# Outputs beside the next unit's state products, running sums after the second products, k and q in two sets of buffers

## What is computed

```python
f = 1.0 / (1.0 + np.exp(-f_logit))
for t in range(S):
    state = f[:, :, t, :, None] * state + np.einsum('bhd,bhe->bhde', k[:, :, t], v[:, :, t])
    y[:, :, t] = np.einsum('bhd,bhde->bhe', q[:, :, t], state)
...
for e in range(E):
    h = np.maximum(x @ w1[e], 0.0)
    out += p[:, e:e + 1] * (h @ w2[e])
```

## Time and profile before

| what | us |
|---|---|
| runs | 1072.81, 1073.47, 1073.48 (median 1073.47) |
| profiled execution, its own time | 1073.53 |
| its span, first to last instruction | 1071.8 |
| busy TensorE matmuls | 1023.2 |
| busy VectorE | 357.1 |
| busy ScalarE | 278.5 |
| busy GpSimd | 87.9 |

### The profile page before, as it was taken

One profiled execution on the slowest core, in us unless ns is written; L12 is line 12 of the kernel. 1 busy time (PEld: TensorE's weight loads), 2 busy tenths in 40 slices (PEclk: granted clock), 3 DMA queues, 4 the chain that ended last, 5 costly groups with the idle time before them and its releaser, 6 DMA issues.

```text
span 1071.8 us, 17708 instructions
## 1 busy us (share of the span) xinstructions
PE 1023.2 (95%) x6997; PEld 959.6 (90%) x6997; DVE 357.1 (33%) x773; ACT 278.5 (26%) x577; POOL 87.9 (8%) x109
## 2 busy tenths in 40 slices
PE   6599999999999999999999999999999999999895
PEld 5488888888889899999999999999999999999542
DVE  5445454554644222222222222222222222222323
ACT  4343333233332331111114111111222222222322
POOL 1240100001000230000005000000230000000000
PEclk9699999999999999999999999999999999999898
DMA  8622343323420330000000300000030004020694
GB/s 182 150 62 57 69 79 70 62 57 69 83 59 15 124 118 1 0 0 0 0 1 1 117 0 0 0 0 0 0 118 1 1 1 177 0 78 2 218 351 177
DMA packets 129761, 67.04 MB, mean 63 GB/s; under 512 B 106656, under 2 KB 125088, under 8 KB 129696
## 3 DMA queue, kind: packets, MB, share of 16 engines
q1 hardware_dynamic: 129696, 66.18, 22.3%
HBM read 56.72 MB, written 4.72 MB: 57 GB/s over the span
## 4 chain that ended last, share of the span: by engine, by line
PE 90%; SPq 5%; DVE 2%; issue 1%; ACT 1%; DMA 0%; DVEq 0%; ACTq 0%
PE ph L1253 13%; PE ph L1255 12%; PE po L1272 12%; PE ph L1254 12%; PE po L1271 12%; PE po L1270 12%; PE pair L1205 2%; PE pc L1229 2%; PE pair L1173 1%; PE pc L1234 1%; PE po L1417 1%; PE ph L1402 1%; PE pc L1213 1%; PE pair L1185 1%; PE pair L1175 1%
## 5 line engine op out<-in xcount | busy, mean ns | idle before, releaser
L980 DVE SCALAR_TENSOR_TENSOR h_lo<-ph,h_hi 128x384 fp32r<-128x384 f32 x256 | 142.7, 557 | 503.4 <-ACT h_hi L747 502.6
L747 ACT ACTIVATE h_hi<-ph 128x384 fp32r<-128x384 f32 x256 | 126.0, 492 | 563.6 <-PE ph L1255 563.6
L1253 PE MATMUL ph<-xT,w_hi 128*128 128x384 f32 (+1 forms) x768 | 266.4, 347 | 2.2 <-DVE xT L961 2.2
L1270 PE MATMUL po<-w_hi,h_hi 128*128 128x384 f32 x768 | 259.2, 338 | 0.0
L1255 PE MATMUL ph<-xT,w_lo 128*128 128x384 f32 (+1 forms) x768 | 257.3, 335 | 0.0
L1272 PE MATMUL po<-w_hi,h_lo 128*128 128x384 f32 x768 | 257.1, 335 | 0.0
L1254 PE MATMUL ph<-xT,w_hi 128*128 128x384 f32 (+1 forms) x768 | 256.9, 335 | 0.0
L1271 PE MATMUL po<-w_lo,h_hi 128*128 128x384 f32 x768 | 256.7, 334 | 0.0
L1253 PEld LDWEIGHTS ph<-xT,w_hi 128*128 128x128 f32 x768 | 144.2, 188 | 8.8 <-issue 4.7
L1254 PEld LDWEIGHTS ph<-xT,w_hi 128*128 128x128 f32 x768 | 144.4, 188 | 0.0
L1270 PEld LDWEIGHTS po<-w_hi,h_hi 128*128 128x128 f32 x768 | 144.2, 188 | 0.1
(11 more groups left out here) (169 smaller groups left out, 701.9 us busy)
## 6 DMA issues: line engine op xcount, KB each, us to landing
v<-in_moe_w_dram SPq DMA_DIRECT2D x15, 1536.0 KB, 10.5
raw<-in_moe_w_dram SPq DMA_DIRECT2D x8, 1536.0 KB, 8.9
f_in<-in_f_logit_dram SPq DMA_DIRECT2D x48, 96.0 KB, 2.6
k_in<-in_k_dram SPq DMA_DIRECT2D x48, 96.0 KB, 2.6
q_in<-in_q_dram SPq DMA_DIRECT2D x48, 96.0 KB, 2.7
v_in<-in_v_dram SPq DMA_DIRECT2D x48, 96.0 KB, 2.6
out_dram<-out_sb SPq DMA_DIRECT2D x5, 768.0 KB, 5.9
x_raw<-yT SPq DMA_DIRECT2D x48, 72.0 KB, 2.2
```

The source lines that it names most:

```text
L747: a.activation(h_hi[:, f % 2, :], ph[f % 2][:, 0:BLK], ACT.Relu).then_inc(h_hi_done, 1)
L980: d.scalar_tensor_tensor(out=h_lo[:, f % 2, :], in0=ph[f % 2][:, 0:BLK], scalar=0.0, in1=h_hi[:, f % 2, :].bitcast(F32), op0=ALU.max, op1= ...
L1253: t.matmul(bank, wh, xh, start=(kk == 0), stop=False, skip_group_check=True)
L1270: t.matmul(bank, hh, w2_hi[:, f, :], start=(f == 0), stop=False, skip_group_check=True)
```

## The change

The state products become a step of their own, P, right behind S. The outputs of a unit stand behind the P of the next unit, in one group of column-wise matmuls; only the last unit of each half has its outputs in its own iteration. C and D move one piece earlier, behind the second piece after the scores. The order of an iteration is now: T, piece, [G], S, P, [Y of the unit before], [W], piece, [X], [L], C or D, piece, [Y of this unit, if it is the half's last], piece. The state products are written to free columns of the pair banks, the running sums to the bank of the outputs. k_in, q_in and qT have two buffers throughout. The opening names P separately and keeps its order otherwise.

```diff
 OPENING = (
-    "G0 L0 G1 C0 D0 L1 T0 T1 S0 S1 C1 D1 Y0 Y1 T2 T3 G2 L2 S2 S3 Y2 Y3 C2 D2 "
-    "W0 W1 T4 G3 S4 L3 X0 W2 Y4 C3"
+    "G0 L0 G1 C0 D0 L1 T0 T1 S0 P0 S1 P1 C1 D1 Y0 Y1 T2 T3 G2 L2 S2 P2 S3 P3 Y2 Y3 C2 D2 "
+    "W0 W1 T4 G3 S4 P4 L3 X0 W2 Y4 C3"
 )
...
         steps.append(("S", u, None))
+        steps.append(("P", u, None))
+        if u > LAG and u % PER_HALF:
+            steps.append(("Y", u - 1, None))
...
-        steps.append(pieces[n + 2])
-        steps.append(("Y", u, None))
         if m + 1 < UNITS // 2:
             steps.append(("D" if u % 2 else "C", m + 1, None))
+        steps.append(pieces[n + 2])
+        if u % PER_HALF == PER_HALF - 1:
+            steps.append(("Y", u, None))
         steps.append(pieces[n + 3])
...
+        def products_of(u, c):
+
+            at_col = BLK + (c if c < BT - 1 else 0) * D
+            return pair_of(u)[:, 0 if c < BT - 1 else 1, at_col:at_col + D]
+
         def sums_bank(m, part):
-            return ph[part] if m <= 2 else bT
+            return ph[part] if m <= 2 else bST
+
+        def before_y(u):
+
+            return 0 if u < LAG else min(u + 3, 2 * QUADS)
...
                 m = u // 2 + 3
-                if m < QUADS and m > 2:
+                if m < QUADS:
                     sp.wait_ge(c_filled, 2 * (m - 1))
                     sp.wait_ge(log_summed, 2 * (m - 1))
                     load_f(m)
-                m -= 1
-                if 2 < m < QUADS:
-                    sp.wait_ge(kd_done, 2 * m)
-                    sp.wait_ge(qd_done, 2 * m)
+                    sp.wait_ge(kd_done, 2 * (m - 1))
+                    sp.wait_ge(qd_done, 2 * (m - 1))
                     load_kq(m)
-                    load_v(m)
+                if 2 < m - 1 < QUADS:
+                    load_v(m - 1)
...
@@ VectorE, scores(u) @@
-                dve.wait_ge(s_filled, u + 1)
+                dve.wait_ge(p_filled, u + 1)
+                at_least(dve, y_filled, before(u) + 1)
...
@@ TensorE, log_sums(m, part), m > 2 @@
-                    pe.wait_ge(s_masked, 2 * (m - 1) + part + 1)
+                    u = 2 * (m - 1) + part
+                    pe.wait_ge(y_taken, u + 1 if u < LAG else u)
+                    pe.wait_ge(c_taken, 2 * m + part)
...
@@ TensorE, turn(u) @@
                 at_least(pe, s_masked, before(u) + 1)
+                at_least(pe, st_done, st_count(before(u) + 1))
...
-                if m >= 2:
-                    pe.wait_ge(c_taken, 2 * m + i + 2 if m + 1 < QUADS else 2 * QUADS)
...
@@ TensorE, outputs(u) @@
                 pe.wait_ge(s_masked, u + 1)
                 pe.wait_ge(st_done, st_count(u + 1))
+                at_least(pe, y_taken, before(u) + 1)
+                at_least(pe, c_taken, before_y(u))
```

More of the change, by code:

```diff
@@ L158, in build @@
     v_in.append(at("v_in2", [P, BT, QC], F32, r_x2 + NT // 2 * DM * 4))
-    k_in = [small_at(first, "k_in0", [P, BT, QC]), small_at(second, "k_in1", [P, BT, QC])]
-    q_in = [small_at(first, "q_in0", [P, BT, QC]), small_at(second, "q_in1", [P, BT, QC])]
+    late_slot = [r_x2 + (NT - 2 * BT) * DM * 4]
+    k_in = [small_at(first, "k_in0", [P, BT, QC]), small_at(late_slot, "k_in1", [P, BT, QC])]
+    q_in = [small_at(first, "q_in0", [P, BT, QC]), small_at(late_slot, "q_in1", [P, BT, QC])]
+    assert late_slot[0] <= r_x2 + (NT - BT) * DM * 4
     f_in = [small_at(first, "f_in0", [P, BT, QC])]
@@ L187, in build @@
     kT = [small("kT0", [P, BLK]), small_at(second, "kT1", [P, BLK])]
-    qT = [small("qT0", [P, BLK]), small_at(second, "qT1", [P, BLK])]
+    qT = [small(f"qT{i}", [P, BLK]) for i in range(2)]
     masked = [small("masked0", [P, 2, BT, P]), small_at(second, "masked1", [P, 2, BT, P])]
@@ L282, in build @@
         qT_done = sem("qT_done")
-        s_filled = sem("s_filled")
         p_filled = sem("p_filled")
@@ L360, in loaded @@
             return 16 * BT * (m // 2 + 1)
-        def kq_of(m):
-            return 1 if m == 1 else 0
         def v_of(m):
@@ L537, in load_kq @@
                 for c in range(BT):
-                    sp.dma_start(k_in[kq_of(m)][:, c].rearrange("p (h d) -> p h d", d=D),
+                    sp.dma_start(k_in[m % 2][:, c].rearrange("p (h d) -> p h d", d=D),
                                  k_dram[b, BT * late + c, :, h0:h0 + QH]).then_inc(kq_landed[m % 2], 16)
                 for c in range(BT):
-                    sp.dma_start(q_in[kq_of(m)][:, c].rearrange("p (h d) -> p h d", d=D),
+                    sp.dma_start(q_in[m % 2][:, c].rearrange("p (h d) -> p h d", d=D),
                                  q_dram[b, BT * late + c, :, h0:h0 + QH]).then_inc(kq_landed[m % 2], 16)
@@ L712, in turn @@
                 act.wait_ge(q_turned, u + 1)
-                a.activation(qT[set_of(u)][:], pair_of(u)[:, 1, 0:BLK], ACT.Copy).then_inc(qT_done, 1)
+                a.activation(qT[u % 2][:], pair_of(u)[:, 1, 0:BLK], ACT.Copy).then_inc(qT_done, 1)
             def outputs(u):
@@ L872, in by_head @@
                 def by_head(t):
-                    return t[kq_of(m)][:, c0:c1].rearrange("p c (h d) -> p (c h) d", d=D)
+                    return t[m % 2][:, c0:c1].rearrange("p c (h d) -> p (c h) d", d=D)
                 n = 2 * m + part + 1
@@ L898, in scores @@
                 s = set_of(u)
-                dve.wait_ge(s_filled, u + 1)
+                dve.wait_ge(p_filled, u + 1)
+                at_least(dve, y_filled, before(u) + 1)
                 d.tensor_tensor(masked[s][:], pair_of(u)[:, :, 0:BLK].rearrange("p a (c t) -> p a c t", t=P),
                                 causal[:].unsqueeze(1).unsqueeze(1).broadcast_to([P, 2, BT, P]), ALU.mult).then_inc(s_masked, 1)
-                dve.wait_ge(p_filled, u + 1)
-                bank = last_of(u)
                 for c in range(BT):
@@ L908, in scores @@
                         rows = slice(WIN * hh, WIN * (hh + 1))
-                        new = bank[rows, c * D:(c + 1) * D]
+                        new = products_of(u, c)[rows, :]
                         into = carry[rows, r, hh, :] if c == BT - 1 else st[s][rows, c, hh, :]
@@ L1204, in scores, with products @@
                         rows = slice(WIN * hh, WIN * (hh + 1))
[L1205 to L1208, removed]
+                        mm = t.matmul(banks[:, hh, cols], kT[s][rows, cols], qT[u % 2][rows, cols], start=True, stop=True)
+            def products(u):
+                m, i = divmod(u, 2)
                 pe.wait_ge(v_landed[v_of(m)], v_loaded(m))
@@ L1212, in scores @@
                         head = 2 * i + hh
-                        mm = t.matmul(bank[WIN * hh:WIN * (hh + 1), c * D:(c + 1) * D], kd[m % 2][:, c, head, :],
+                        mm = t.matmul(products_of(u, c)[WIN * hh:WIN * (hh + 1), :], kd[m % 2][:, c, head, :],
                                       v_in[v_of(m)][:, c, head * D:(head + 1) * D], start=True, stop=True)
@@ L1233, in outputs @@
                             state = st[s][:, c - 1, hh, :] if c else carry[:, r, hh, :]
-                            mm = t.matmul(bank[WIN * hh:WIN * hh + D, cols], state, qT[s][:, cols],
+                            mm = t.matmul(bank[WIN * hh:WIN * hh + D, cols], state, qT[u % 2][:, cols],
                                           start=False, stop=True, skip_group_check=True)
@@ L1264, in sums @@
                     pe.wait_ge(y_taken, 4)
+                    pe.wait_ge(st_done, st_count(4))
                 if f == 0:
@@ L1284, in _ @@
                     scores(i)
+                elif kind == "P":
+                    products(i)
                 elif kind == "Y":
```

## The result

The changed kernel takes 1081.87 us (median of 4, 1081.32 to 1082.27) against 1073.21 (median of 4, 1072.81 to 1073.48): ratio 1.0073, 95% interval 1.006 to 1.0085. It is slower. On another chip later it took 1080.69 against 1073.45, ratio 1.0059, interval 1.0045 to 1.0074.

The account below looks back on a forecast made before the run. TensorE, busy for 1023.2 of 1071.8 us, was taken to bound the kernel. Stage +4.0, opening +5.0 and clock +3.4 made +12.4 us on 1073.53: 1086, range 1075 to 1094.

Parts of the forecast that it names:

- The chain at a half's end: Outputs of unit 4k+3 to scores of unit 4k+5, 16.25 us: TensorE newly waits 2.6 us, six times, 15.6 us.
- The wait of T: T's 0.51 us wait for late k and q after D disappears at 13 places: 6.6 us won.
- The switches of the array: Outputs directly behind state products save an entry and exit of 0.10 us each for 20 units: 4.0 us won.
- Net of the stage: First stage: new half-end waits less existing waiting, T's waits and array switches, +4.0 us without clock falls.
- The opening: Before the first h: earlier quad 3 loads and running sums waiting for the yT copy cost +5.0 us.
- The clock in the waits: At the six half-end waits: two falls to TensorE's lower clock level at 1.7 us each, +3.4 us.
- faster: Rival: the wait before the scores of unit 4k+5 does not become real, 1065 to 1067 us; chance 0.13.
- half-way: Rival: the half-end chain is 1 to 1.5 us shorter each time than counted, 1073 to 1079 us; chance 0.15.
- the fourth: Rival: T keeps its waits because kT or the adds hold it, +6.6 us, 1089 to 1096; chance 0.10.
- The first, waits without a clock fall: Rival: half-end waits appear but TensorE's clock holds, 1082.5 us, from 1080 to 1084; chance 0.20.
- the likeliest case: The forecast itself: half-end waits with one to six clock falls, 1084 to 1094 us, 1086 likeliest; chance 0.42.

Follow-up runs that it names:

- e1: Changed kernel with the count of `y_final` ahead of the twelve loads on SyncE's queue instead of behind them: 1063.86 us, ratio 0.9905.
- e7: Kernel before the change, with only the count of `y_final` moved ahead of the loads on SyncE's queue: 1073.98 us, ratio 0.9999.
- e8: Kernel before the change, with C and D one piece earlier and the count of `y_final` ahead of the loads: 1068.28 us, ratio 0.9942.
- e2: Changed kernel with the k and q loads of quad 3 back behind the rows of unit 3: 1077.77 us, ratio 1.0032.
- e3: Changed kernel with quad 3's k and q loads late and its first running sums in the old bank: 1076.74 us, ratio 1.0021.
- e9: Changed kernel with the count of `y_final` ahead of the loads, run again on another occasion: 1062.62 us, ratio 0.9885.
- e5: The changed kernel itself, unedited, run again beside the kernel before: 1080.69 us, ratio 1.0059.
- e6: Changed kernel with `y_final` counted ahead of the loads, quad 3's loads late and its first running sums in the old bank: 1061.34 us, ratio 0.9883.

## Why the prediction was right

Slower was forecast, 1086.0 with 1075 to 1094; measured 1081.87. By its own steps:

- **The chain at a half's end** was right in place: kT releases the scores, and e1 removes the waits by touching SyncE's order alone. Its size was off twice. I counted six half ends; there are five, since behind unit 27 the changed `next_loads` finds only v to load (the k and q of the last quad are already there), and the chain of half 6 is short. And I took its 16.25 us from one half end, the tightest of the six. There the chain is 16.30 us after the change; at the other four it is 15.6 to 16.0, which is 0.4 to 0.8 us less than the same distance in the kernel before. That is at least in part slack in the chain, which the distance to the scores does not show: behind unit 19 it was 16.56 us before and is 15.73 after, and before the change VectorE stood idle within it for 0.61 us (row below). TensorE's own work between the two was sized well (13.65 forecast, 13.5 to 13.7 in e1). The wait is thus 2.3 us in the mean against 2.6, and 11.3 us in all in place of 15.6.

```profile
231.85 0.56 DVE L883 TENSOR_TENSOR kd<-kd,k_in 128x384 f32<-128x384 f32 x1 [0.61 <-ACT kd L708]
```

- **The wait of T**: 6.6 forecast, 6.4 measured (e7 to e8). In the kernel before, the h piece to T takes 2.2 us at twelve of the 13 places and 1.81 at the last; in e8 it is 1.7 at every one.
- **The switches of the array**: 4.0 forecast, 6.9 measured (e8 to e1), the mis-sized term on the side of the gain. Summed over A to B, the products are 2.0 us shorter, the outputs 0.7 and the pieces h and s 4.2. I had priced the gap before and behind the outputs, 0.10 us each, and not the 0.11 us by which the expert piece after such a switch is itself longer (1.67 us where it is else 1.56): 21 more pieces have their usual length in e1.
- **Net of the stage**: +4.0 and 3.4 for the clock forecast, -0.2 measured: 11.3 of waits, 1.6 for one clock fall and 0.3 for the end of the opening's low stretch, against 13.4 of gains (306.40 to 292.96 in e1). Without the clock it is about -2, so this part of the forecast had the wrong sign.
- **The opening**: +5.0 forecast, +4.7 measured at the first h; x_high at 53.20 (forecast 53.2), sums at 55.80 (55.85), first h at 59.66 (59.7), at the lower clock as assumed. e2 and e3 confirm both its causes.
- **The clock in the waits**: two falls forecast, one in each of the two profiles. The fall behind a half end cost 1.6 us in the first profile, and another 3.8 us of clock came from behind C, which I had not forecast at all. Without its clock terms the forecast was +9.0 us; the first profile without its own is +3.4, the second +4.1. So the direction follows from the opening and the waits, but that the total came within 4 us of 1086 is in good part luck.
- **The rivals**: the waits are real, so "faster" falls; the chain is at most 0.6 us shorter than counted, not 1 to 1.5, so "half-way" falls as it was told; T's waits are gone, so the fourth falls. The first, waits without a clock fall, 1080 to 1084, contains the measured 1081.87, which lies below the 1084 to 1094 of the likeliest case. By the profile neither describes it: there is one fall at a half end, and smaller waits than both assume.

## What to carry to other kernels

When work is moved past a point where another engine's chain ends, compare the chain's length with the work that is left over it: here it was filled to 0.2 us at the tightest half end and had 0.4 to 0.8 us to spare at the others, and 2.6 us moved away came back as 2.0 to 2.8 us of idle time. So measure it at every place where it occurs, and look for idle time within it: by that much it can shrink. Then look in the chain for what need not stand there. Twelve loads ahead of a semaphore count cost nothing before, and after the change 11.3 us of the first stage, 13.2 with the clock; with the count ahead of them the same change is about 1% faster than the kernel before (ratios 0.9905 and 0.9885).

## What the runs showed of the hardware

TensorE's clock fell to the lower level behind some waits of 1.9 to 2.1 us and not behind others of the same length: behind 8 of the 20 half-end waits in the four profiles that have them (1, 1, 4 and 2 of five), and nowhere between A and B in the eight profiles without (e9's 0.9 us at A are the end of the opening's low stretch). The wait of 2.2 us at B, which all twelve profiles have, was followed by a low stretch of 3.4 us in five of them (e1, e2, e5, e8 and e9). One such stretch costs 1.6 us: from B to C it is 648.81 us in e1 and 647.23 in e6.
